# A routed attention and expert kernel: the fullest expert of two batches goes first, and its first slot is computed while the routing is still worked out

## The reference

```python
# attention: B, H, S, D = 4, 8, 576, 64; softmax attention mixed with a memory read
out = g * (phi(q) @ M) / (phi(q) @ z + 1e-6) + (1 - g) * softmax(q k^T / 8, causal) @ v
x = out.transpose(0, 2, 1, 3).reshape(2304, 512)
# mixture of 8 experts, the fullest logit takes the token
e_idx = argmax(x @ w_gate)
y = gate_w * sigmoid(x @ w_output_gate)[e_idx] * (relu(x @ w1[e_idx]) @ w2[e_idx])   # 512 -> 1024 -> 512
# second stage, every token: 512 -> 2048 -> 512
h = y @ w_in;  result = (h - tanh(h)) @ w_out
```

## Time and profile before

| | us |
|---|---|
| median of 3 runs (1021.72 to 1023.37) | 1022.81 |
| profiled execution | 1023.92 |
| its span | 1022.1 |
| PE busy in the span | 994.2 (97%) |
| end of the last gate products | 271.42 |
| first matmul of slot 0, of slot 1 | 292.23, 302.76 |
| mean slot afterwards | 12.3 |

### The profile page before, as it was taken

How to read it: one execution, slowest core, us unless ns; L and a number is a source line. 1 busy time by engine, 2 the same in 40 slices (tenths; PEclk the granted TensorE clock), 3 DMA queues, 4 the chain that set the end, 5 groups by cost and what they waited for, 6 DMA issues and landing times.

```text
span 1022.1 us, 16780 instructions
## 1 busy us (share of the span) xinstructions
PE 994.2 (97%) x5474; PEld 818.4 (80%) x5475; DVE 644.7 (63%) x1238; ACT 501.0 (49%) x1043; POOL 469.1 (46%) x332
## 2 busy tenths in 40 slices
PE   7999999999989999999999999999999999999998
PEld 4667667676558888888888879999999999999997
DVE  4687675877734444444444439777777777777664
ACT  5777687786243120022112046565565555655653
POOL 3565586775589651067337147332232322322221
PEclk8999999999899999999999999999999999999999
DMA  9466575531577351165391210010010110100000
GB/s 212 120 161 170 156 208 171 149 98 39 199 265 289 124 188 59 57 215 179 123 362 48 82 35 29 1 56 8 1 62 1 30 34 1 49 14 1 32 1 31
DMA packets 51009, 103.66 MB, mean 101 GB/s; under 512 B 7424, under 2 KB 16640, under 8 KB 50432
## 3 DMA queue, kind: packets, MB, share of 16 engines
q1 hardware_dynamic: 34176, 55.96, 18.8%
q10 hardware_dynamic: 13856, 37.42, 10.2%
q0 software_dynamic: 2912, 9.44, 2.9%
HBM read 82.62 MB, written 20.19 MB: 101 GB/s over the span
## 4 chain that ended last, share of the span: by engine, by line
PE 75%; DVE 5%; POOL 4%; issue 1%; ACT 1%; ACTq 0%; DVEq 0%; POOLq 0%
PE scores L1470 6%; PE scores L1472 6%; PE scores L1471 6%; PE average L1424 5%; PE average L1426 4%; PE average L1425 4%; PE scores L1413 4%; PE scores L1412 4%; PE scores L1411 4%; PE average L1487 2%; PE mix L1488 2%; PE turned L1487 2%; PE average L1488 2%; PE mix L1487 2%; PE turned L1488 2%; PE average L1486 2%
## 5 line engine op out<-in xcount | busy, mean ns | idle before, releaser
L577 POOL TENSOR_TENSOR g_lo<-g,g_hi 128x384 fp32r<-128x384 f32 x96 | 98.1, 1022 | 273.8 <-ACT g_hi L786 273.3
L540 POOL TENSOR_TENSOR ring<-ring 128x2048 fp32r<-128x2048 f32 x30 | 137.3, 4604 | 104.9 <-ACT ring L725 104.9
L725 ACT ACTIVATE ring<-ring 128x2048 fp32r<-128x2048 f32 x30 | 55.7, 1907 | 178.8 <-PE scores L1413 81.7
L1470 PE MATMUL scores<-yt_hi,w_in_hi 128*128 128x384 f32 x384 | 131.2, 342 | 1.7 <-DVE yt_lo L1155 1.7
L1472 PE MATMUL scores<-yt_hi,w_in_lo 128*128 128x384 f32 x384 | 129.5, 337 | 0.0
L1471 PE MATMUL scores<-yt_lo,w_in_hi 128*128 128x384 f32 x384 | 128.8, 335 | 0.0
L776 ACT ACTIVATE sq<-scores 128x384 f32<-128x384 f32 x96 | 47.2, 491 | 164.4 <-PE scores L1472 164.4
L1147 DVE COPY_PREDICATED ser<-big,th 128x384 f32<-128x384 int32 x96 | 119.1, 1241 | 3.3
L1142 DVE TENSOR_TENSOR ser<-ser,sq 128x384 f32<-128x384 f32 x96 | 55.8, 581 | 96.1 <-ACT ser L779 96.1
L603 ACT ACTIVATE prob<-scores,nmx 128x128 f32<-128x128 f32 (+3 forms) x128 | 66.3, 524 | 44.9 <-DVE nmx L864 42.8
L1411 PE MATMUL scores<-ring,xt_hi 128*128 x200 | 80.5, 402 | 3.5 <-POOL ring L540 1.8
(11 more groups left out here) (270 smaller groups left out, 2499.9 us busy)
## 6 DMA issues: line engine op xcount, KB each, us to landing
ring<-in_w ACTq DMA_DIRECT2D x13, 2048.0 KB, 9.0
q_sb<-in_qt SPq DMA_DIRECT2D x46, 288.0 KB, 4.1
k_sb<-in_kt SPq DMA_DIRECT2D x32, 288.0 KB, 4.2
xin<-x_sorted SPq DMA_DIRECT2D x27, 256.0 KB, 3.0
y_sorted<-y_sb SPq DMA_DIRECT2D x25, 256.0 KB, 2.2
v_sb<-in_v SPq DMA_DIRECT2D x16, 256.0 KB, 2.8
ring<-in_w SPq DMA_DIRECT2D x8, 512.0 KB, 4.0
...
```

The source lines that it names most:

```text
L540: pool.tensor_tensor(ring[:, ring_at(k), 1, part], ring[:, ring_at(k), 1, part].bitcast(F32), ring[:, ring_at(k), 0, part].bitcast(F32), A ...
L577: pool.tensor_tensor(g_lo[:, t % GRING, :], g32[:, t % 2, :], g_hi[:, t % GRING, :].bitcast(F32), ALU.subtract).then_inc(g_lo_ok, 1)
L1470: mm(ff_h(t), w_h, yt_hi[:, j % 2, c, :], start=c == 0, stop=False)
```

## The change

**Order of experts.** In the third quarter of batch 1's routing the count also gives how many tokens each expert has so far. DVE takes the largest (`largest`, in pair 11) and writes the new order (`order`, in pair 12): that expert, then the others as before. For these inputs it is expert 5, so the slots by expert are 3, 1, 2, 3, 6, 2, 1, 4. SP loads this expert's two matrices in pieces in pairs 12 and 13. Every later use of an expert's number on a queue is a register load from `order_i` (`expert_of`), also ahead of each zero fill.

**Split of units 0 and 1.** ACT rounds all 16 eighths in pairs 14 to 16 (`HIGH`). POOL forms the rest of unit 0 in pairs 14 and 15, and DVE that of unit 1: five eighths after the attention, three after the slots' first rows are in the table.

**Slot 0.** Its 128 rows are all from batches 0 and 1 and are loaded as soon as the scores are done. PE turns them in pair 16, begins `up` ahead of the last count, ends it behind the count, and then runs the whole `down` of slot 0 before slot 1's `up`, with three short runs of idle products (4, 5, 5) in place of the 60.

**Unit 2 and the rest.** Unit 2 is loaded after the rows of slots 1 and 2 instead of at the end of attention; units 3 and 4 wait for unit 2; POOL's units begin with unit 2, still behind `r_tails`. Slots 1 to 6 are written out ahead of the loop.

```diff
+AT_FIRST = (4, 5, 5)
+CHOICE = 1
+PEELED = 7
+HIGH = {(14, 0): (0,), (14, 1): (1,), (14, 2): (2,), (14, 3): (3,), (15, 0): (4, 5), (15, 1): (6, 7), (15, 2): (8,), (15, 3): (9,),
+        (15, 4): (10,), (16, 0): (11, 12), (16, 1): (13, 14, 15)}
...
-        def fill(queue, e):
+        def expert_of(queue, k):
+            return queue.value_load(order_i[0:1, k // 2:k // 2 + 1], min_val=0, max_val=E - 1)
+        def fill(queue, j):
+            e = expert_of(queue, 2 * j)
+            row = queue.value_load(fill_i[0:1, bass.ds(e, 1)], min_val=0, max_val=E * REG)
...
-            sp.wait_ge(x_ok, NP * QT)
-            load_unit(sp, 2)
+            row = sp.value_load(first_i[0:1, 0:1], min_val=0, max_val=E * REG)
+            sp.wait_ge(q_split, NP)
+            sp.wait_ge(scored, NP * QT)
+            sp.dma_start(xin[:, 0, :], xs[bass.ds(row, P), :]).then_inc(xin_ok[0], 16)
...
-            sp.wait_ge(r_table, 1)
+            sp.wait_ge(r_slots, 1)
...
-            for k in range(XIN):
+            for k in range(1, XIN):
                 load_x(k, k)
+            sp.wait_ge(x_ok, NP * QT)
+            load_unit(sp, 2, expert_of(sp, 2))
...
+            pool.wait_ge(first_lo, 2)
+            pool.sem_inc(part_lo, 2)
             pool.wait_ge(r_tails, 1)
-            for k in range(1, UNITS):
+            for k in range(2, UNITS):
...
             act.wait_ge(x_ok, NP * QT)
-            for k in range(1, 3):
-                convert(k)
             act.wait_ge(scattered, 16 * TILES)
-            act.wait_ge(xin_ok[0], 16)
-            load_unit(act, 3)
-            load_unit(act, 4)
+            act.wait_ge(w_ok[ring_at(2)], landed(2))
+            load_unit(act, 3, expert_of(act, 3))
+            load_unit(act, 4, expert_of(act, 4))
+            convert(2)
...
+            def largest():
+                rs(dve.tensor_reduce(first_s[:, 0:1], n_first[:, :], AX.X, ALU.max))
+                rs(dve.scalar_tensor_tensor(n_first[:, :], n_first[:, :], first_s[:, 0:1], expert_f[:, :], ALU.is_equal, ALU.mult))
+                rs(dve.tensor_reduce(first_s[:, 1:2], n_first[:, :], AX.X, ALU.max))
...
+            def first_low(q):
+                r, part = ring_at(1), slice(q % 8 * EIGHTH, (q % 8 + 1) * EIGHTH)
+                dve.wait_ge(early_hi, q + 1)
+                last = dve.tensor_tensor(ring[:, r, 1, part], ring[:, r, 1, part].bitcast(F32), ring[:, r, 0, part].bitcast(F32), ALU.subtract)
...
+                        if i == 2 and n == NP:
+                            turn_in(0, 0)
```

353 lines of the change are left out of this document (233 added, 120 removed).

## The result

| | kernel before | changed kernel |
|---|---|---|
| median | 1023.31 us (1021.40 to 1025.05, 16 runs) | 1021.70 us (1019.31 to 1023.90, 16 runs) |
| ratio | | 0.9982, 95% interval 0.9974 to 0.9990 |
| profiled execution, time and span | 1023.92, 1022.1 | 1021.86, 1020.0 |

The change makes the kernel 1.8 us faster (0.0018 x 1023.3) where 3.7 were forecast. A second comparison of the two gave 0.9993 (0.9980 to 1.0006), which alone would not tell the two kernels apart. The sign was right; the time lies in the range. All ratios here are over executions within 1.5% of the fastest of their kernel, which leaves out a single one, of e6, that took 5429 us.

The account below looks back on a forecast made before the run. PE, DVE and ACT bound attention in turn and PE the slots, so gains lie between. Terms: -5.2 + 1.5 = -3.7 us, from 1023.92 to 1020.2, on the median's scale 1019.1 us; range 1015.0 to 1023.6.

Parts of the forecast that it names:

- Attention, +1.65 to L: Attention: gate products end 1.65 us later, 1.2 for `largest` and `order`, 0.45 for slot 0's turn; eighths taken as 0.
- L: Mark: end of the gate products, 271.42 us in the profile before; forecast 273.1 after the change.
- From C to slot 1: Between last count and slot 1: table rows at C + 10.9, down(0) done at C + 15.6, slot 1's rows landed at C + 15.9.
- C: Mark: end of the last count, forecast at 275.9 us.
- U1: Mark: first matmul of slot 1, forecast at C + 18.4 = 294.3 us, against 302.76 before.
- the charge of 1.5 for the clock: Clock falls at the count's matmuls (1.2) and inside down(0) or ahead of slot 1 (1.8): 1.5 of 3.0 us charged.
- POOL: Ahead of slot 4: POOL starts behind `r_tails` at U1 + 12.6 = 306.9, then six halves take 27.4 us.
- Slot 4: Start of slot 4's `up`: forecast 334.4 us, set by POOL, against 339.64 before; 5.2 us won at the full clock.
- From there PE takes 12.3 us for each slot: From slot 4 on: PE's time per slot expected the same, 12.3 us, after the change as before.
- Rival 2: Zero fills: every added register load takes 0.92 us, slot 1's rows come 2.8 later; 0.9 won, 1021.9 us; chance 0.19.
- rival 3: Slots 0 and 1: lower clock throughout, up to 6.8 us slower, 1025.6 for 40 to 45 matmuls; chance 0.14 with another rival.
- Rival 1: Attention and clock: DVE's steps hide and neither fall comes; 6.8 us won, 1016.0 us; chance 0.17.

Follow-up runs that it names:

- e6: Changed kernel with the fullest expert written as the constant 5 and `largest` left out; ratio to the kernel before 0.9978.
- e15: Kernel before, unchanged, profiled once more; 752.1 us from the end of the gate products to the end.
- e16: Changed kernel, unchanged, run again; 748.1 us from the end of the gate products to the end, ratio to the kernel before 0.9993.
- e7: Changed kernel with one register load per zero fill instead of two, and unit 1's three late eighths on POOL; ratio to the kernel before 0.9971.
- e1: Changed kernel with 20 idle products on PE ahead of slot 4's first product; ratio to the kernel before 0.9953.
- e4: Changed kernel with unit 1's three late eighths done by POOL instead of DVE; ratio to the kernel before 0.9986.
- e10: Changed kernel with the small-step tail ahead of slot 1, unit 2 loaded behind slot 0's rows, units 3 and 4 once slot 1's rows landed; ratio to kernel before 0.9877.

## Why the prediction was right in sign and wrong in size

*Attention, +1.65 to L.* Right: 1.4 between the matched e15 and e16. Of it `largest` and `order` are 1.8 (forecast 1.2), the pairs that the eighths left gave back 0.4 in each of two intervals (16.36 for 16.76, 16.33 for 16.78), and the pair that they went to lost 0.6 (17.75 for 17.20); two earlier intervals changed by -0.25 and +0.17 (14.28 for 14.53, 16.49 for 16.32), 1.4 in all. In the first pair of profiles L even came 0.4 sooner, since the kernel before had two more falls of the clock, which say nothing of the change.

*From C to slot 1.* U1 = C + 18.4 was forecast; 21.7 came in the first profile and 19.3 to 21.7 in the eight with the same code, so the sum was short by 1 to 3 us, of which the charge of 1.5 for the clock covers a part. Two terms were mis-sized. The fills: `r_fill` came at C + 0.7 as I had it, but the last fill was issued at C + 11.0 and not 9.45, since a fill cost about 2.6 us and not 2.2, and all had landed at C + 14.3 instead of 12.5. This did not decide the first profile, where down(0) came last: the splits of slot 0 waited longer for PE (table rows at C + 12.8 for 10.9; in the eight profiles 10.2 to 12.8), and down(0)'s second half ran behind the eighths and at the lower clock, so that the turn began at C + 19.4. e7 shows what was left in one profile with both cured, C + 18.3. What makes the table's rows come at 10.2 in one execution and at 12.8 in another of the same code is not shown.

*POOL.* U1 + 12.6 was forecast for `r_tails`, 12.4 measured (307.63 - 295.22); 27.4 for six halves, 27.31 measured. PE waited 1.1 us ahead of slot 3 and 5.6 ahead of slot 4, where 1 to 2 and about 6 stood.

*Slot 4.* From L to slot 4: 68.2 before less 5.4 (the sum without attention, with the clock) is 62.8 forecast, 64.1 and 63.5 measured. Against the profile from which I predicted that is 4.1 and 4.7 won, against the three profiles of the kernel before (mean 69.1) 5.3. That the last is the forecast value is in part luck: slot 1 came later than my sum, and two of the three have the fall at slot 1, of 1.6 us each, that the first lacks and of which I knew nothing.

*The step that failed* is "From there PE takes 12.3 us for each slot", together with the charge for the clock. I forecast PE's wait of about 6 us ahead of slot 4, wrote that an idle PE loses its clock, put a price on two such places, and none on the longest one. It costs 2.4 us by the rows of slot 4 and 2.6 by e1, which is the gain that was missing: -5.3 + 2.5 + 1.4 = -1.4, and the comparisons gave -1.8 +- 0.8 and -0.7 +- 1.3.

*The rivals.* Rival 2 (the fills decide) held half: the fills were slower than forecast and hold slot 1 as soon as down(0) does not, as in e4. Of rival 3 only the sign of the clock's part came: three falls, of which two had idle ahead of them (2.29 and 5.62 us) and the first none to speak of, and never one through a whole slot. Rival 1 took less idle behind the gate products as a reason that the first fall might stay away; it came in every profile, even with no idle at all (e10).

What remains open is why falls in attention and at the gate products come at different places from one execution to the next in identical code; those in attention move a single profile by up to 2.6 us. The runs show only that they do. The port as the cause of the long steps of DVE was not tried apart from these runs either.
